# Rows of x kept on chip through attention and stored in eight transfers; a third buffer for the fold's chunks; routing's loads in another order

## What is computed

```python
# attention, r, k, v: (4, 8, 768, 48)
for t in range(S):
    kt, vt, rt = (k[:, :, t], v[:, :, t], r[:, :, t])
    cur = np.einsum('bhd,bhe->bhde', u[None] * kt, vt)
    y[:, :, t] = np.einsum('bhd,bhde->bhe', rt, state + cur)
    state = w[None, :, :, None] * state + np.einsum('bhd,bhe->bhde', kt, vt)
# mixture of experts on x (3072, 384)
do_compute = x @ w_skip > 0
e_idx = np.argmax(xc @ w_gate, axis=1)
y[mask] = gate_w[mask, None] * (np.maximum(xc[mask] @ w1[e], 0.0) @ w2[e])
out[do_compute] = xc + y
# gated layers
h = (x @ w1) * (x @ w2) @ w3
return h @ w_out
```

## Time and profile before

| | us |
|---|---|
| median of three runs | 635.29 |
| the profiled execution | 633.52 |
| its span, first to last instruction | 631.7 |
| TensorE busy in the span | 603.7 (96%) |
| VectorE, ScalarE, GpSimd busy | 295.6, 215.9, 149.4 |

### The profile page before, as it was taken

The page is one execution under the profiler, slowest core; times in us unless marked ns, Lnnn a source line. Parts: engine busy times, 40 slices in busy tenths (PEclk is TensorE's granted clock), DMA queues, the critical chain, the costliest instruction groups (busy, mean ns, idle before and its releaser), DMA issues. The chain is left out here.

```text
span 631.7 us, 17461 instructions
## 1 busy us (share of the span) xinstructions
PE 603.7 (96%) x7377; PEld 536.2 (85%) x7377; DVE 295.6 (47%) x456; ACT 215.9 (34%) x383; POOL 149.4 (24%) x183
## 2 busy tenths in 40 slices
PE   7699898799999999999999999999999999999997
PEld 6699887756799998999878888898898889888886
DVE  6478778368177886777222232232132214123222
ACT  2244444325355565545141232132122213123212
POOL 7467677325113444441150000000000000000000
PEclk9899999799999999999999999999999999999999
DMA  7689999574366665773140020002002001001001
GB/s 137 119 170 186 185 185 210 167 265 163 111 239 223 217 223 203 266 270 119 33 138 1 1 100 1 1 36 65 0 1 101 0 1 50 1 1 50 1 0 51
DMA packets 103801, 67.77 MB, mean 107 GB/s; under 512 B 79252, under 2 KB 97816, under 8 KB 103760
## 3 DMA queue, kind: packets, MB, share of 16 engines
q1 hardware_dynamic: 75824, 57.88, 30.4%
q10 hardware_dynamic: 26144, 4.74, 4.0%
q0 software_dynamic: 1792, 4.58, 2.0%
HBM read 55.92 MB, written 12.19 MB: 108 GB/s over the span
## 5 line engine op out<-in xcount | busy, mean ns | idle before, releaser
L1527 DVE TENSOR_TENSOR gl_g_sb<-gl_a_sb,gl_pab 128x512 f32<-128x512 f32 x48 | 33.0, 688 | 186.3 <-ACT gl_a_sb L1504 186.3
L1447 PE MATMUL gl_pab<-gl_xT_hi,wm_lo 128*128 128x512 f32 x288 | 112.9, 392 | 0.0
L1447 PE MATMUL gl_pab<-gl_xT_lo,wm_hi 128*128 128x512 f32 x288 | 112.8, 392 | 0.0
L1447 PE MATMUL gl_pab<-gl_xT_hi,wm_hi 128*128 128x512 f32 x288 | 112.2, 389 | 0.0
L1504 ACT ACTIVATE gl_a_sb<-gl_pab 128x512 f32<-128x512 f32 x48 | 28.8, 599 | 183.9 <-PE gl_pab L1447 183.9
L1447 PEld LDWEIGHTS gl_pab<-gl_xT_hi,wm_lo 128*128 128x128 f32 x288 | 54.0, 188 | 11.4
L1447 PEld LDWEIGHTS gl_pab<-gl_xT_hi,wm_hi 128*128 128x128 f32 x288 | 54.1, 188 | 10.6 <-DVE gl_xT_lo L1534 0.3
L1447 PEld LDWEIGHTS gl_pab<-gl_xT_lo,wm_hi 128*128 128x128 f32 x288 | 54.0, 188 | 10.5
L1213 PE MATMUL ex_ph<-ex_xT_hi,ew_w_hi 128*128 128x224 f32 x192 | 52.9, 275 | 0.0
L1310 DVE TENSOR_TENSOR ew_w_lo<-ew_w_in,ew_w_hi 128x768 fp32r<-128x768 f32 x32 | 45.1, 1409 | 16.6 <-ACT ew_w_hi L1272 15.6
L1213 PE MATMUL ex_ph<-ex_xT_hi,ew_w_lo 128*128 128x224 f32 x192 | 52.7, 274 | 0.0
(11 more groups left out here) (203 smaller groups left out, 1215.7 us busy)
## 6 DMA issues: line engine op xcount, KB each, us to landing
w_in<-in_moe_w SPq DMA_DIRECT2D x8, 1536.0 KB, 9.2
ew_w_in<-in_moe_w SPq DMA_DIRECT2D x8, 1536.0 KB, 6.7
w_in<-in_moe_w SPq DMA_DIRECT2D x14, 512.0 KB, 7.2
k_in<-in_k SPq DMA_DIRECT2D x48, 96.0 KB
v_in<-in_v ACTq DMA_DIRECT2D x48, 96.0 KB, 3.4
r_in<-in_r SPq DMA_DIRECT2D x48, 96.0 KB
xbuf<-x_nat SPq DMA_DIRECT2D x24, 192.0 KB
w_in<-xbuf SPq DMA_DIRECT2D x12, 384.0 KB, 4.0
```

The source lines that it names most:

```text
L1447: m = pe.matmul(p_ab[f % 2][w][:, :], a[:, w * KD + k, cols], b[t.slot][:, k, :], start=(k == 0 and n == 0), stop=(k == KD - 1 and n == 2))
L1527: dve.tensor_tensor(g_sb[f % 2][:, :], a_sb[f % 2][:, :], p_ab[f % 2][1][:, :], ALU.mult).then_inc(s_g, 1)
```

## The change

- `store`, its waits and the wait at the end of attention's SP list are gone. ScalarE gets a new part, `keep`: for each tile it copies x(t-2) from `x_nat` into `x_all`, which holds all 24 tiles (two tensors of 128 x 12 x 384). `x_out` now waits for `keep` of four tiles back instead of the store.
- `x_all` lies where `wm_hi` and `wm_lo` (weights that only the experts' stage fills) lie later; those two are now allocated after attention.
- `store_x` stores from `x_all`, one transfer for each batch: chunks 0 to 4 (960 KB each) at the end of attention's SP list, when `keep` has done 20 tiles, and chunk 5 (192 KB each) in routing. Nothing in attention waits for them; the first gather in routing waits on GpSimd for all eight.
- The fold has three buffers for chunks of w3, so chunk 2 is loaded at the end of attention, before the stores. Routing's SP list is now: chunk 3, the last four stores, chunk 4, w1, chunks 5 and 6, w2, chunk 7.

```diff
--- before.py
+++ after.py
@@ -50,15 +50,15 @@
         self.w3T = [sb(f"w3T{i}", [P, self.KF, P]) for i in range(3)]
         self.wo = sb("wo", [P, self.KF, DM])
         self.wf = sb("wf", [P, self.KF, DM])
-        self.s_w3 = [sem(f"fold_w3{i}") for i in range(2)]
+        self.s_w3 = [sem(f"fold_w3{i}") for i in range(3)]
         self.s_wo = [sem(f"fold_wo{i}") for i in range(2)]
         self.s_T, self.s_Tout = sem("fold_T"), sem("fold_Tout")
         self.s_W, self.s_Wout = sem("fold_W"), sem("fold_Wout")
     def load(self, sp, chunks):
         for i in chunks:
-            wait(sp, self.s_T, i - 1)
-            sp.dma_start(self.w3_in[i % 2][:, :], self.w3[i * P:(i + 1) * P, :]).then_inc(self.s_w3[i % 2], 16)
+            wait(sp, self.s_T, i - 2)
+            sp.dma_start(self.w3_in[i % 3][:, :], self.w3[i * P:(i + 1) * P, :]).then_inc(self.s_w3[i % 3], 16)
     def load_w_out(self, sp):
         for h in range(2):
@@ -67,10 +67,10 @@
     def turn(self, pe, i, banks):
-        wait(pe, self.s_w3[i % 2], 16 * (i // 2 + 1))
+        wait(pe, self.s_w3[i % 3], 16 * (i // 3 + 1))
         wait(pe, self.s_Tout, 2 * i)
         for g in range(self.KF):
-            m = pe.transpose(banks[g // 4][:, (g % 4) * P:(g % 4 + 1) * P], self.w3_in[i % 2][:, g * P:(g + 1) * P], self.ident[:, :])
+            m = pe.transpose(banks[g // 4][:, (g % 4) * P:(g % 4 + 1) * P], self.w3_in[i % 3][:, g * P:(g + 1) * P], self.ident[:, :])
         m.then_inc(self.s_T, 1)
     def turned(self, act, i, banks):
@@ -99,6 +99,16 @@
         wait(act, self.s_W, i + 1)
         act.activation(self.wf[:, i, :], bank[:, 0:self.DM], ACT.Copy).then_inc(self.s_Wout, 1)
+
+
+def store_x(sp, env, xbuf, c, chunks, s_stored):
+
+
+    B, S, HALF = env["batch"], env["seq"], P // 2
+    for b in range(B):
+        rows = xbuf[b * S + c * P:b * S + (c + chunks) * P, :]
+        sp.dma_start(rows.rearrange("(g s) w -> s g w", s=HALF),
+                     env["x_all"][b // 2][b % 2 * HALF:(b % 2 + 1) * HALF, 2 * c:2 * (c + chunks), :]).then_inc(s_stored, 16)
 def attention(nc, env, r, k, v, w, u, xbuf):
@@ -147,6 +157,7 @@
         bonus = [sb(f"bonus{i}", [P, H]) for i in range(2)]
         v_bonus = [sb(f"v_bonus{i}", [P, H, D]) for i in range(2)]
         x_nat = [sb(f"x_nat{i}", [P, 2, W]) for i in range(2)]
+        x_all, s_stored = env["x_all"], env["s_stored"]
         xT = [sb(f"xT{i}", [P, 2, KC, C]) for i in range(2)]
         state = [sb(f"state{i}", [P, 2, HP, DP]) for i in range(2)]
         state_sum = [sb(f"state_sum{i}", [P, 2, HP, D]) for i in range(2)]
@@ -169,7 +180,7 @@
         s_rkin = [sem(f"s_rkin{i}") for i in range(NS)]
         s_vin = [sem(f"s_vin{i}") for i in range(NS)]
-        s_store = [sem(f"s_store{i}") for i in range(2)]
+        s_kept = sem("s_kept")
         s_kdec, s_kT, s_Tr, s_rT = (sem(n) for n in ("s_kdec", "s_kT", "s_Tr", "s_rT"))
         s_S, s_mask, s_U, s_Y, s_YT = (sem(n) for n in ("s_S", "s_mask", "s_U", "s_Y", "s_YT"))
         s_own, s_nat, s_x, s_xTp, s_xT = (sem(n) for n in ("s_own", "s_nat", "s_x", "s_xTp", "s_xT"))
@@ -252,21 +263,12 @@
                     sp.dma_start(u_all[:, :, :].rearrange("p h d -> p (h d)"),
                                  u.rearrange("h d -> (h d)").unsqueeze(0).broadcast_to([P, W])).then_inc(s_u, 16)
-            def store(t):
-                if t.a == 0:
-                    return
-                wait(sp, s_x, t.done())
-                for jj in range(2):
-                    sp.dma_start(xbuf[bass.ds(t.chunk(P, (2 * t.pr + jj) * S), P), :].rearrange("(a s) w -> s a w", a=2), x_nat[t.pr][half(jj), :, :]).then_inc(s_store[t.pr], 16)
-
-            def extra(c, j, f):
-                if f is store and at(c, j, NT - NS):
-                    fold.load(sp, [0])
-                    fold.load_w_out(sp)
-                    fold.load(sp, [1])
-            schedule(sp, ((load_rk, 4), (store, -2)), 4, 2, extra)
-            for i in range(2):
-                sp.wait_ge(s_store[i], 32 * NCH)
+            schedule(sp, ((load_rk, 4),), 4, 0)
+            fold.load(sp, [0])
+            fold.load_w_out(sp)
+            fold.load(sp, [1, 2])
+            wait(sp, s_kept, BASE + NS * env["early"])
+            store_x(sp, env, xbuf, 0, env["early"], s_stored)
         @block.tensor
         def _(pe):
@@ -428,7 +430,7 @@
             def issue_v(t, halves):
                 for jj in halves:
                     act.dma_start(v_in[half(jj), t.slot, :, 0:D], v[2 * t.pr + jj, :, bass.ds(t.chunk(P, C * t.a), C), :].rearrange("h s d -> s h d")).then_inc(s_vin[t.slot], 16)
-            for x in (s_kT, s_YT, s_xT, s_scaled[0]):
+            for x in (s_kT, s_YT, s_xT, s_scaled[0], s_kept):
                 act.sem_inc(x, BASE)
             for x in s_vin:
                 act.sem_inc(x, 32)
@@ -464,6 +466,10 @@
                 wait(act, s_xTp, t.done())
                 act.activation(xT[t.pr][:, :, :, :].rearrange("p j q c -> p j (q c)"), p_K[:, :, HALF:HALF + KC * C], ACT.Copy).then_inc(s_xT, 1)
+            def keep(t):
+                wait(act, s_x, t.done())
+                act.activation(x_all[t.pr][:, bass.ds(t.chunk(2, t.a), 1), :], x_nat[t.pr][:, t.a, :].unsqueeze(1), ACT.Copy).then_inc(s_kept, 1)
+
             def logits_out(c):
                 return act.activation(lg_parts[:, bass.ds(c * LW, LW)].rearrange("p (g x) -> p g x", g=2), p_Y[:, :, HALF:HALF + LW // 2], ACT.Copy)
@@ -480,7 +486,7 @@
                     act.wait_ge(s_Y, BASE + NT + 1)
                     logits_out(NCH - 1).then_inc(s_lg, 1)
                     fold.turned(act, 1, [p_R[:, i, :] for i in range(2)])
-            schedule(act, ((kT_out, 1), (xT_out, -2), (new_state, -1), (load_rest, 2), (load_v, 3), (y_out, 0)), 1, 3, extra)
+            schedule(act, ((kT_out, 1), (xT_out, -2), (new_state, -1), (keep, -2), (load_rest, 2), (load_v, 3), (y_out, 0)), 1, 3, extra)
         @block.vector
         def _(dve):
@@ -531,7 +537,7 @@
             def x_out(t):
                 wait(dve, s_nat, t.done())
                 wait(dve, s_vb, t.done())
-                wait(dve, s_store[t.pr], t.chunk(32))
+                wait(dve, s_kept, t.done(-NS))
                 dve.tensor_tensor(x_nat[t.pr][:, t.a, :].rearrange("p (g h d) -> p g h d", g=2, d=D),
                                   p_R[:, :, HALF:2 * HALF].rearrange("p g (h d) -> p g h d", d=DP)[:, :, :, 0:D],
                                   v_bonus[t.pr][:, :, :].rearrange("p (g h) d -> p g h d", g=2), ALU.add).then_inc(s_x, 1)
@@ -739,11 +745,13 @@
         with nc.Block(no_gpsimd_drain=True) as block:
             @block.sync
             def _(sp):
-                fold.load(sp, [2])
+                fold.load(sp, [3])
+                store_x(sp, env, xbuf, env["early"], NT // 4 - env["early"], env["s_stored"])
+                fold.load(sp, [4])
                 ex.load_w1(sp, 0)
-                fold.load(sp, [3])
+                fold.load(sp, [5, 6])
                 ex.load_w2(sp, 0)
-                fold.load(sp, [4, 5, 6, 7])
+                fold.load(sp, [7])
             @block.gpsimd
             def _(pool):
@@ -767,6 +775,7 @@
                 pool.wait_ge(s_slot, 1)
                 slot_values(pool, 2, piece[:, 0, :], s_gval)
                 pool.wait_ge(s_table, 1)
+                pool.wait_ge(env["s_stored"], 2 * 16 * env["batch"])
                 for i in range(2):
                     ex.gather(pool, xbuf, 0, i, env["slot_token"][0:ex.rows(i), i:i + 1])
                 for i in range(1, 3):
@@ -1570,7 +1579,8 @@
             "ident": ident, "s_iota": s_iota, "n_logits": E + 1,
             "w_gate": moe_w_gate, "w_skip": moe_w_skip, "wm": (moe2_w1, moe2_w2),
             "fold": Fold(nc, sb, sem, ident, s_iota, moe2_w3, moe2_w_out),
-            "s_wmlo": sem("s_wmlo"), "lg": sb("lg", [P, E + 1, N // P]), "seq": S,
+            "s_wmlo": sem("s_wmlo"), "lg": sb("lg", [P, E + 1, N // P]), "seq": S, "batch": B,
+            "s_stored": sem("s_stored"), "early": 5,
             "slot_token": sb("slot_token", [P, NSL], I32),
             "slot_gate": sb("slot_gate", [P, NSL]),
             "n_over": sb("n_over", [P, 1], I32),
@@ -1578,14 +1588,20 @@
             "pad1": sb("pad1", [P, (2 * LINE - sum(-(-4 * n // 32) * 32 for n in ((E + 1) * N // P, NSL, NSL, 1, NO))) // 4]),
             "s_scattered": [sem(f"s_scattered{i}") for i in range(2)], "n_scattered": E // 2,
-            "wm_hi": sb("wm_hi", [P, 2 * KD, FM], F32R),
-            "wm_lo": sb("wm_lo", [P, 2 * KD, FM], F32R),
         }
         env["tables"] = Tables(*scope(c, "tb_"), N // P, E, NSL, CAP, ROOM, NO, S)
         sb("pad2", [P, (LINE - TABLE_BYTES % LINE) // 4])
         env["p_pair"] = c.enter_context(nc.psum_tensor("p_pair", [P, 2, 512], F32))
-        attention(nc, env, r, k, v, w, u, xbuf)
+
+
+        with ExitStack() as cx:
+            sbx, _ = scope(cx)
+            env["x_all"] = [sbx(f"x_all{i}", [P, S // (P // 2), DM]) for i in range(2)]
```

(4 more changed lines are left out.)

## The result

The changed kernel takes 630.7 us (median of 20 runs, 628.6 to 634.5) where the kernel before takes 634.4 (20 runs beside it, 630.0 to 637.6): a ratio of 0.9943, 95% interval [0.9923, 0.9962]. That is 3.7 us of the 10.3 that I forecast, and the time lies 0.2 us above the upper end of my range. The profiled execution spans 628.4 us against 631.7.

A forecast was written before the change was run, and what follows sets the result against it. TensorE is busy 603.7 of 631.7 us, so only its idle and half-clock time could be had. Gains 4.5 + 2.8 + 3.0 + 0.3 - 0.3 = 10.3 us take the median from 635.3 to 625.0; range 621 to 630.5.

The forecast's parts named there:

- (1): Attention's rounds: without store waits and stores in SP's round, the three later ones match the first's 15.35 us; 4.5 us less.
- second rival: Attention's rounds don't shorten because DMA transfers pace them; only the tail gains, 629.5 us; chance 0.16.
- (2): Attention's tail: tile 21's `x_out` no longer waits for its store, so TensorE's 2.8 us of idle time go.
- (3): Attention's tail: without the idle time TensorE keeps full clock from 118 to 125 us; 3.0 us gained.
- (6): Large stores at attention's end: 350 GB/s, done near 118 us, w1 and first gather covered; they cost nothing.
- third rival: Attention's tail: the clock falls all the same, so the gain of (3) is lost, 628.0 us; chance 0.10.
- (4): Routing: chunk 2 is on chip before it begins, so TensorE's turn needn't wait for the load; 0.3 us gained.
- (5): ScalarE in attention: `keep` adds 24 ACTIVATEs of about 0.48 us, mostly hidden; 0.3 us lost in all.
- fourth rival: Attention's rounds: `keep` makes ScalarE the bound and delays each YT; 640 us; chance 0.10.
- (7): Routing: chunks 3 to 7 load later but at least one product ahead of use, w2 also later; no cost.
- the last 0.06: Remaining chance: transfers come late after all, giving 642 us or more.

The follow-up runs named there:

- experiment 5: Changed kernel with stores back in the rounds, two per pair of tiles out of `x_all`, nothing waiting, no large stores: 629.1 us, 0.9921 of the kernel before.
- the version: Changed kernel, stores split: one sixth after 20 kept tiles, three behind chunk 0's turn, two late in routing; GpSimd's slot values earlier: 624.8 us, again 625.8.
- experiment 7: Changed kernel with all large early stores held until TensorE has turned chunk 0: 628.1 us, 0.9902 of the kernel before.
- experiment 9: Changed kernel with no stores in attention, all of them in routing behind chunk 3: 637.5 us, 1.0039 of the kernel before.
- experiment 2: Changed kernel with three instead of five chunks in the early stores, issued sooner, the rest in routing: 629.4 us, 0.9917 of the kernel before.
- experiment 6: Kernel before with only the third buffer, chunk 2 loaded in attention and routing's new load order; stores unchanged: 634.5 us, 1.0009 of the kernel before.
- experiment 1: Changed kernel with the four early stores held until TensorE has turned chunk 1: 632.4 us, 0.9974 of the kernel before.
- experiment 3: Changed kernel with early stores for two batch entries instead of four, the others stored in routing: 629.9 us, 0.9943 of the kernel before.
- experiment 4: Changed kernel with 32 more warm-up transposes at the start, shifting TensorE's later code by 64 instructions: 636.2 us, 1.0028 of the kernel before.

## Why the prediction missed, step by step

**(1) The rounds.** Right: 46.48 us for the last three against 46.05, a gain of 4.1 instead of 4.5. That both the waits and SP's issuing pace them was argued from SP's timeline; experiment 5 puts 1.9 us on the waits and 2.2 on the stores in SP's list, their issue and their transfer together. The second rival, in which the rounds don't shorten, falls.

**(2) and (3), the tail.** The 2.8 us of idle time went, as forecast, and where the stores keep out of the way the tail takes 19.5 to 20.2 us against 18.8 by my sum, with clock 1.00 (both runs of the version and experiment 7). That the full clock follows from the missing idle time alone is not shown: it fell in experiment 9 and a second time in experiment 2 without one. In the changed kernel the tail gained nothing, because step (6) was wrong. The third rival (the clock falls all the same) is half of what happened: it fell, but behind a new idle time, and that idle time cost more than the one removed. Against the 19.50 us of the version, the changed kernel's two tails are 6.0 and 7.5 us longer: 3.8 and 4.2 by the stall. The rest is 2.3 and 3.2. In the first trace 0.4 of it lies ahead of the stall; what is left, 1.9 and 3.2, is TensorE at half clock behind it.

**(4) Chunk 2.** Right, and a little small: 0.55 us in routing instead of 0.3, and no DMA wait before the turn. I did not see that in the kernel before the same load would lengthen a wait for a store (experiment 6); it does no harm once nobody waits for stores.

**(5) `keep`.** Small, as I had it. It takes 0.51 to 0.54 us instead of 0.48. If all of the 0.15 us by which a round is longer than my 15.35 is its cost, that is 0.6 us in four rounds, against my 0.3; nothing shows that it is, and in experiment 5, with `keep` in it, the first round takes 15.11 us. The fourth rival falls.

**(6) The stores.** This step failed, in "the stores cost nothing", and its first error is in "350 GB/s is my estimate at full share". That figure came from a window of loads. In the changed kernel only stores move from 110 to 124 us, at 205 to 325 GB/s by windows of 2 us and 243 on average, with a share of 0.95 to 1.01 until 122; in experiment 7 it was 217. SP issues them at 106.3 and not behind chunk 2 at 99.8, since it waits 6.5 us for `keep` of tile 19, a wait that my sum left out. So the 3.9 MB take 18 us from there instead of 11, and end near 124 and not near 118. Done by 118, they would still have filled the DMA engines at 113 to 114, when the code lands in a quiet tail. So the larger error is what I left out: I asked only which data stands behind the stores, and not that code comes through the same DMA engines. That code was late is what the runs show: TensorE stood still for 3.77 and 4.24 us, the stall shrank with the stores (experiments 1 and 3) and moved with the count of instructions (experiment 4). What I said of w1 and the first gather held: neither waited for a transfer. Experiments 1, 3, 7 and 9 show where that cover ends.

The Trainium skill ("Runtime: NRT & Kernel Launch", section "Instruction fetch mechanics") says that a sequencer's code is refilled in blocks of 16 KiB, 256 instructions, by a DMA queue of its own, and that the cost of a boundary is mostly hidden. The first half agrees with the 0.02 MB packets and with the exact shift of experiment 4. "Mostly hidden" holds in experiment 1, where the packet landed 4 us ahead of its use; with the DMA engines full of stores it landed 5 to 6 us later than that, and nothing hid it. The Trainium skill's "DMA: Bandwidth & Descriptors", section "Issuing engines are not separate DMA queues", says that transfers started by the scalar, sync or gpsimd engine run on the same 16 DMA engines. It does not say so of the queue that brings code; the late packet here says that this queue has no engines to itself either.

The signs were there in the trace of before. In the ramp, from 14 to 29 us, it has four stalls of 0.7 to 2.1 us that read "issue" in the middle of a group of like matmuls, and a code packet lands ahead of each:

```profile
24.53 0.29 PE L317 MATMUL p_Y<-w_gates,xT 64*64 64x9 f32 x6 [2.08 <-issue]
```

I read the dip of the clock there as waiting for the first tiles. There are no large stores in the ramp, and the last of the four stalls, 1.48 us up to 28.95, comes with the DMA engines nearly idle (a share of 0.34 from 26 to 28 us and 0.00 behind it). So stores are what makes the code late in the tail, but not the only thing that can.

**(7)** Right: routing takes 35.47 to 35.49 us in six kernels, whatever else they change.

The chances: 0.70 for faster by over 1% was too much. Three of the rivals took a part of my sum away or put a cost on `keep`, and the last 0.06 were for transfers that come late; none let the stores hold up TensorE in the tail, the one part of the change whose price I had only by estimate. That the time came out only 0.2 us above the range is luck: it lies close to the 629.5 and 628.0 of the second and third rivals, and neither is what happened.

## What to carry to other kernels

Before a large transfer is put where "nothing waits for it", ask what comes through the same DMA engines during its whole length, at the rate measured for its own direction and shape: the loads, and the engines' code, wherever straight-line code is being entered for the first time. An idle time marked "issue" inside a group of identical instructions, with a packet of the instruction queue landing shortly before it ends, is that case; shifting the program by a few dozen instructions shows it. And a transfer's issue is work too: four large stores kept SP busy for 6.5 us, which matters as soon as a barrier stands behind it.
